# GpSimd's weight splits of a fused attention and MLP kernel, taken out from between four attention pairs and put behind them in larger groups

## Chip, cores and metric
The kernel runs on one core of a Trainium2 chip. The metric is the device time of one execution in microseconds (us). The time before is 1022.74 us, the median of 3 runs (1019.49 to 1027.27).

## What is computed
Attention over 4 batches, 8 heads, 576 positions, 64 channels, then two MLPs on the 2304 rows of 512 values that it gives. All data is float32.

```python
def _attn_ref(q, k, v):
    # downsampled by 4, softmax attention, repeated 4 times
    out_up = np.repeat(out_d, factor, axis=2)
    # local: |i - j| < 4
    scores = np.where(mask, scores, -1000000000.0)
    ...
    return (out_up + out_local).astype(np.float32)
def _moe_ref(x, w_in, w_out):
    h = x @ w_in
    g = h * np.cos(h)
    return (g @ w_out).astype(np.float32)
# then _moe2_ref: RMS norm, (silu(xn @ w_gate) * (xn @ w_val)) @ w_out
```

## The kernel before
**Work and its order.** Two heads form a pair, so that a batch has four attention pairs (PAIRS = 4). The rows are worked on in 6 chunks of 384. Batch 0's attention runs alone ("Wide", with several buffers); the attention of batches 1 to 3 ("Narrow", one buffer each) is spread by hand over the steps of the first MLP's chunks 0 to 2. Each engine has its own program, written out in order; they meet at semaphores.

**The first MLP and its weights.** A weight unit is a tile of 128x512 values. The first MLP has 32 of them (U1 = 32), the even ones for the product up (L984 to L986 with 384 columns), the odd ones for the product down (the same lines with 512 columns). TensorE multiplies in float32r; for accuracy each weight is split in a high part and the rest. ScalarE makes the high part of the first 16 units (U_EARLY = UP * PAIRS = 16, line L527, four after each pair of batch 0). GpSimd makes everything else: the high part of units 16 to 31 (L423) and the rest of all units (L425). Its function `split_unit` waits for the load, makes the high part if `hi_here` is true, waits for it, and makes the rest. Step f of a chunk on TensorE (`chunk1`, steps 0 to 18) needs unit 2f at its head for up(f) and unit 2(f - 3) + 1 for down(f - 3) later in the step.

**GpSimd's order.** For each pair j of batch 0: `value_sums` (sums of 4 rows of v: L399 and L404, once for each of the two heads), `normalise` twice (softmax times the reciprocal: L411 on the local part, L414 on the downsampled one), then four splits (units 4j to 4j + 3). Then `batch(1, (5, 5, 5, 1))`: for each pair of batch 1 the same sums and normalisations, and behind them 5, 5, 5 and 1 splits, units 16 to 31. Batches 2 and 3 have no splits.

**What waits for GpSimd.** TensorE's `transposes` of a pair (L937, L940) need `probs_ready`, which L414 gives. Its `values` (L953, L961) need `vd_ready` of L404. The next load of GpSimd's own operand, vg, stands in SyncE's queue behind a wait for `vd_ready`: the load for the second head of a pair is issued only when L404 of the first head is done. Behind it in the same queue stand the load of vw (L331), in pairs 0 and 1 of batch 1 that of a weight group (L335), and the load of the next pair's qk (L319).

**Places of batch 1's pairs on TensorE.** PE_WHERE gives, for each pair, the step and half of six pieces (scores of head 0, local scores of head 1, downsampled scores of head 1, transposes of head 0, of head 1, values). A half of 0 is behind up(step), one of 1 behind down(step - 3):

```python
    PE_WHERE = (((1, 0), (2, 0), (3, 0), (4, 0), (4, 1), (5, 0)),
                ((5, 1), (6, 0), (6, 1), (7, 1), (8, 0), (8, 1)),
                ((9, 0), (9, 1), (10, 0), (11, 1), (12, 0), (12, 1)),
                ((13, 0), (13, 1), (14, 0), (15, 0), (16, 0), (16, 1)))
```

**The other engines.** VectorE in batch 0: maxima and differences (L684, L691, L697, L699), sums and reciprocals (L710, L713, L717), copies of the transposed downsampled part (`copy_ptd`, L722), the four-row sums of q and k (L663), the addition of both attention parts into XY (`add_up`, L672). Before chunk 0, ScalarE copies a column third of x into the high part xs (L538) and VectorE makes its rest (L747). In the chunks VectorE has L779, L781, L787 and L751 for each f, ScalarE L570, L576, L578 and L547. On TensorE, the masks are L897 to L900, local scores L903, downsampled scores L920.

Of the kernel before, what the change touches and what calls it, by code (L numbers as in the profile page):

```python
# [31 lines left out]
U1, U2 = 2 * F1, 3 * F2  # L32
UP = 4
U_EARLY = UP * PAIRS
BANK = 12
GU = 4
QT = SD // 2
# [36 lines left out]
def attention_and_two_mlps(nc, qk, vwin, vgrp, w1, w2, rms_g, const, out):  # L74

    def at(name, shape, dtype, offset):
        return nc.alloc_sbuf_tensor_at(name, shape, dtype, offset=offset)
# [7 lines left out]

    W = [at(f"W{i}", [P, BANK, 2, 512], F32R, slots_at + i * BANK * 4096) for i in range(U2 // BANK)]
    W_raw = [at(f"W_raw{i}", [P, BANK, 2, 512], F32, slots_at + i * BANK * 4096) for i in range(U2 // BANK)]

# [37 lines left out]
    def part(start, end):  # L126
        small[:] = [start, end]
# [4 lines left out]
    buffers = {}  # L132
    for i, slot in enumerate((U1, 2 * BANK)):
        part(slots_at + slot * 4096, slots_at + (U2 if i == 0 else U1) * 4096)
# [54 lines left out]
    def loads(kind, b, j):  # L189

        return 1 if kind is Wide else PAIRS * b - PAIRS + j + 1
# [65 lines left out]
    def raw_of(bank, i):  # L257

        return W_raw[bank][:, bass.ds(i, 1), 1, :].rearrange("p o n -> p (o n)")

    def part_of(bank, i, part):

        return W[bank][:, bass.ds(i, 1), part, :].rearrange("p o n -> p (o n)")

    def group_of(bank, first):

        return W_raw[bank][:, bass.ds(first, GU), 1, :]

    def w_part(slot, part):
        return W[slot // BANK][:, slot % BANK, part, :]  # L270

# [5 lines left out]
    def y_tile(c, t):  # L277
        return XY[:, bass.ds(c * (TT * 512) + t * 512, 512)]
# [3 lines left out]
    def hold(eng, semaphore, value):  # L282

        eng.wait_ge(semaphore, value)
        if not isinstance(value, int):
            eng.sem_inc(passed, 1)
# [25 lines left out]
    def sync_program(sp):  # L313
# [13 lines left out]
        def load_values(kind, b, j):  # L327
            n = PAIRS * b + j
            if kind is Narrow:
                hold(sp, pv_done, n)  # L330
            sp.dma_start(kind.vw[j][:, :, :], vwin[bass.ds(n, 1)].rearrange("o p a d -> (o p) a d")).then_inc(kind.vw_in[j], 16)  # L331

        def load_group(src, g, slot0, k):

            sp.dma_start(group_of(slot0 // BANK, slot0 % BANK), src[GU * g:GU * g + GU].rearrange("u p n -> p u n")).then_inc(group_in[k], 16)  # L335

# [9 lines left out]
        load_values(Wide, 0, PAIRS - 1)  # L346
        for g in range(PAIRS - 1, 2 * BANK // GU):
            load_group(w1, g, GU * g, g)
# [33 lines left out]
    def pool_program(pool):  # L382
        g = nc.gpsimd
        g.memset(mhalf[:, :], -0.5).then_inc(setup, 1)
        g.memset(ones[:, :], 1.0).then_inc(setup, 1)

        g.memset(rinv[:, :], 1.0).then_inc(rinv_ready, 1)
        hold(pool, setup, 2)
        hold(pool, rinv_ready, 1)

        def value_sums(kind, b, j):

            n = PAIRS * b + j
            for s in range(2):
                vg = kind.vg[j][s]

                hold(pool, kind.vg_in[j], 32 if kind is Wide else 16 * (2 * loads(kind, b, j) - 1 + s))
                g.tensor_tensor(vg[0:QT, :, 0:2, :], vg[0:QT, :, 0:2, :], vg[0:QT, :, 2:4, :], ALU.add).then_inc(vt_ready, 1)  # L399
                hold(pool, vt_ready, 2 * n + s + 1)  # L400
                if kind is Narrow and s == 0:
                    hold(pool, pv_done, n)
                vd = kind.vd[j][:, :, :].rearrange("p (k s) d -> p k s d", s=2)[0:QT, :, s, :]
                g.tensor_tensor(vd, vg[0:QT, :, 0, :], vg[0:QT, :, 1, :], ALU.add).then_inc(vd_ready, 1)  # L404
                hold(pool, vd_ready, 2 * n + s + 1)

        def normalise(kind, b, j, s):
            u = 2 * (PAIRS * b + j) + s
            hold(pool, recip_ready, u + 1)
            p = kind.prob[j][:, s, 0:TP, :]  # L410
            g.tensor_tensor(p, p, recip[:, s, 0:TP].unsqueeze(2).to_broadcast([P, TP, WIN]), ALU.mult).then_inc(local_probs, 1)  # L411
            hold(pool, local_probs, u + 1)
            p = kind.probd[j][0:QT, s]
            g.tensor_tensor(p, p, recip[0:QT, s, TP:TP + 2].unsqueeze(2).to_broadcast([QT, 2, SD]), ALU.mult).then_inc(probs_ready, 1)  # L414
            hold(pool, probs_ready, u + 1)

        def split_unit(slot, order, hi_here=True):

            bank, i = divmod(slot, BANK)
            raw, hi, lo = raw_of(bank, i), part_of(bank, i, 0), part_of(bank, i, 1)  # L420
            hold(pool, group_in[order // GU], 16)
            if hi_here:
                g.tensor_tensor(hi, raw, ones[:, 0:1].to_broadcast([P, 512]), ALU.mult).then_inc(unit_hi, 1)  # L423
            hold(pool, unit_hi, order + 1)
            g.tensor_tensor(lo, raw, hi.bitcast(F32), ALU.subtract).then_inc(unit_ready, 1)  # L425
            hold(pool, unit_ready, order + 1)

        for j in range(PAIRS):
            value_sums(Wide, 0, j)  # L430
            normalise(Wide, 0, j, 0)
            normalise(Wide, 0, j, 1)
            for u in range(UP * j, UP * j + UP):
                split_unit(u, u, hi_here=False)

        def batch(b, units=(0,) * PAIRS):

            first = U_EARLY
            for j in range(PAIRS):
                value_sums(Narrow, b, j)  # L440
                normalise(Narrow, b, j, 0)
                normalise(Narrow, b, j, 1)
                for u in range(first, first + units[j]):
                    split_unit(u, u)
                first += units[j]
            scale_y(b - 1)

        def scale_y(c):

            hold(pool, ssq_ready, TT * c + TT)  # L450
            g.tensor_scalar(msq[:, :], ssq[:, :], 1.0 / DM, 1e-6, ALU.mult, ALU.add).then_inc(ms_ready, 1)
            hold(pool, ms_ready, c + 1)
            g.tensor_tensor(rinv[:, :], msq[:, :], mhalf[:, :], ALU.pow).then_inc(rinv_ready, 1)
            hold(pool, rinv_ready, c + 2)
            for t in range(TT):
                hold(pool, y_copied, TT * c + TT + t + 1)
                g.tensor_tensor(y_tile(c, t), y_tile(c, t), rinv[:, t:t + 1].to_broadcast([P, 512]), ALU.mult).then_inc(y_scaled, 1)

        batch(1, (5, 5, 5, 1))  # L460
        with pool.Fori(2, B) as b:
            batch(b)
        for u in range(GU):
            split_unit(U1 + u, U1 + u)
        with pool.Fori(ACH, NCH - 1) as c:
            scale_y(c)
        for u in range(U1):
            split_unit(u, U2 + u)
        scale_y(NCH - 1)
# [626 lines left out]
    with block as blk:  # L1096
        blk.sync(sync_program)
        blk.gpsimd(pool_program)
        blk.scalar(act_program)
        blk.vector(dve_program)  # L1100
        blk.tensor(pe_program)
# [52 lines left out]
```

## Time and profile before
| what | us |
|---|---|
| median of 3 runs (lowest, highest) | 1022.74 (1019.49, 1027.27) |
| span of the profiled execution | 1022.4 |
| TensorE busy | 991.5 (97%) |
| VectorE busy | 516.8 (51%) |
| ScalarE busy | 426.6 (42%) |
| GpSimd busy | 259.8 (25%) |

The page gives the profiled execution's span, from its first to its last instruction, and no device time of its own; the median of the three runs is 0.3 us above that span. In the rows, PE is TensorE, DVE VectorE, ACT ScalarE, POOL GpSimd and SP SyncE; L425 is line 425 of the kernel. "[0.25 <-DVE probd L722]" says that the engine sat idle for 0.25 us before the row and that VectorE's L722 ended this. PEclk is the granted clock as a share of full speed.

### The profile page before, as it was taken

What the parts mean: (1) busy time and instruction counts of PE and PEld (TensorE: products, weight loads), DVE (VectorE), ACT (ScalarE), POOL (GpSimd) and SP (SyncE); (2) the same over time, 40 slices, a digit from 0 to 9 for tenths busy, and PEclk for the clock granted to TensorE, in tenths of its full rate; (3) what the DMA queues carried; (4) which work ended last, traced back from release to release, by engine and by line L of the source; (5) the groups of instructions that cost most, each with busy time, mean ns of one, the idle gap of its engine ahead of it and who ended that gap; (6) DMA issues with size and microseconds to landing.
All of it is one profiled execution on the core that took longest, in us unless ns stands there. A gap on an engine that the chain in (4) does not pass through costs nothing.

```text
span 1022.4 us, 17445 instructions
## 1 busy us (share of the span) xinstructions
PE 991.5 (97%) x6320; PEld 887.3 (87%) x6320; DVE 516.8 (51%) x1176; ACT 426.6 (42%) x923; POOL 259.8 (25%) x285
## 2 busy tenths in 40 slices
PE   6889999999899999999999999999999999999998
PEld 5677787888788899998997999999999999999997
DVE  6767776676676664554667424324324324324322
ACT  3556566665665665655655213113113113112111
POOL 4947763221422150100299930000000000000000
PEclk9999999999999999999999999999999999999999
DMA  9622111111111100000134000000000000000000
GB/s 275 210 92 92 52 51 54 51 51 52 52 51 51 63 2 1 1 0 0 42 124 135 31 1 1 31 0 0 31 0 0 31 0 0 31 0 0 31 1 31
DMA packets 19208, 43.95 MB, mean 43 GB/s; under 512 B 1616, under 2 KB 1744, under 8 KB 19152
## 3 DMA queue, kind: packets, MB, share of 16 engines
q1 hardware_dynamic: 19152, 43.16, 12.9%
q8 instruction: 40, 0.66, 0.3%
q14 instruction: 16, 0.13, 0.0%
HBM read 38.44 MB, written 4.72 MB: 42 GB/s over the span
## 4 chain that ended last, share of the span: by engine, by line
PE 82%; DVE 6%; ACT 4%; POOL 3%; issue 3%; DMA 1%; DVEq 0%; SPq 0%; POOLq 0%; ACTq 0%
PE ps L984 26%; PE ps L986 25%; PE ps L985 25%; PE ps L903 2%; POOL W L425 1%; DVE ub L781 1%; ACT ub L576 1%; PE ps L920 1%; PE ps L1065 1%; DVE ub L779 1%; ACT ub L578 1%; DMA qk<-qk 1%; DVE XY L672 1%; ACT probd L487 1%; PE ps L937 1%
## 5 line engine op out<-in xcount | busy, mean ns | idle before, releaser
L984 PE MATMUL ps<-xs,W 128*128 128x384 f32 x960 | 327.8, 341 | 1.9 <-DVE xs L747 1.4
L986 PE MATMUL ps<-xs,W 128*128 128x384 f32 x960 | 324.0, 338 | 4.1 <-issue 4.1
L985 PE MATMUL ps<-xs,W 128*128 128x384 f32 x960 | 323.4, 337 | 0.0
L984 PE MATMUL ps<-W,ring 128*128 128x512 f32 x504 | 202.8, 402 | 0.0
L986 PE MATMUL ps<-W,ring 128*128 128x512 f32 x504 | 199.1, 395 | 0.0
L985 PE MATMUL ps<-W,ring 128*128 128x512 f32 x504 | 198.7, 394 | 0.0
L984 PEld LDWEIGHTS ps<-xs,W 128*128 128x128 f32 x960 | 181.4, 189 | 15.6 <-issue 7.6
L985 PEld LDWEIGHTS ps<-xs,W 128*128 128x128 f32 x960 | 181.6, 189 | 4.6
L986 PEld LDWEIGHTS ps<-xs,W 128*128 128x128 f32 x960 | 181.4, 189 | 0.0
L839 DVE TENSOR_TENSOR ub<-ub,ps 128x384 f32<-128x384 f32 x72 | 39.9, 554 | 248.9 <-ACT ub L629 248.9
L629 ACT ACTIVATE ub<-ps 128x384 f32<-128x384 f32 x72 | 35.4, 492 | 270.0 <-PE ps L986 270.0
L986 PEld LDWEIGHTS ps<-W,ring 128*128 128x128 f32 x504 | 94.9, 188 | 20.9
L984 PEld LDWEIGHTS ps<-W,ring 128*128 128x128 f32 x504 | 95.1, 189 | 18.6 <-issue 2.7
L985 PEld LDWEIGHTS ps<-W,ring 128*128 128x128 f32 x504 | 95.2, 189 | 15.8
L425 POOL TENSOR_TENSOR W<-W_raw,W 128x512 fp32r<-128x512 f32 x68 | 91.4, 1343 | 5.3
L787 DVE TENSOR_TENSOR ub<-ub,ps 128x384 f32<-128x384 f32 x96 | 53.0, 552 | 70.2 <-ACT ub L578 70.2
L570 ACT ACTIVATE ub<-ps,consts 128x384 f32<-128x384 f32 x96 | 55.1, 574 | 56.0 <-PE ps L986 54.2
L576 ACT ACTIVATE ub<-ub 128x384 f32<-128x384 f32 x96 | 50.4, 525 | 65.7 <-DVE ub L781 65.7
L635 ACT ACTIVATE ring<-ub 128x384 fp32r<-128x384 f32 x72 | 37.8, 525 | 82.6 <-DVE ub L843 82.6
L779 DVE TENSOR_SCALAR ub<-ub 128x384 f32<-128x384 f32 x96 | 44.7, 466 | 50.5 <-ACT ub L570 50.4
L848 DVE TENSOR_TENSOR ring<-ub,ring 128x384 fp32r<-128x384 f32 x72 | 42.7, 594 | 39.6 <-ACT ring L635 39.6
L751 DVE TENSOR_TENSOR ring<-ub,ring 128x384 fp32r<-128x384 f32 x96 | 60.9, 634 | 2.5 <-ACT ring L547 2.5
(91 smaller groups left out, 1014.5 us busy)
## 6 DMA issues: line engine op xcount, KB each, us to landing
W_raw<-w SPq DMA_DIRECT2D x17, 1024.0 KB, 6.1
qk<-qk SPq DMA_DIRECT2D x14, 576.0 KB, 4.1
vw<-vwin SPq DMA_DIRECT2D x14, 384.0 KB, 3.1
out<-XY SPq DMA_DIRECT2D x18, 256.0 KB, 2.0
vg<-vgrp SPq DMA_DIRECT2D x26, 144.0 KB
qk_more<-qk SPq DMA_DIRECT2D x2, 576.0 KB, 16.1
vg_more<-vgrp SPq DMA_DIRECT2D x6, 144.0 KB
vw_more<-vwin SPq DMA_DIRECT2D x2, 384.0 KB, 15.5
```

What stands on the lines that cost most here:

```text
L425: g.tensor_tensor(lo, raw, hi.bitcast(F32), ALU.subtract).then_inc(unit_ready, 1)
L570: a.activation(v, HB[f % NH], ACT.Identity, scale=INV_2PI, bias=consts[:, 0:1]).then_inc(turns_ready, 1)
L576: a.activation(v, v, ACT.Abs).then_inc(abs_ready, 1)
L635: a.activation(ring[:, f % 3, 0, :], ub[:, f % 2, :], ACT.Copy).then_inc(ahi_ready, 1)
L751: v.tensor_tensor(ring[:, f % 3, 1, :], ub[:, f % 2, :], ring[:, f % 3, 0, :].bitcast(F32), ALU.subtract).then_inc(glo_ready, 1)
L779: v.tensor_scalar(w, w, MAGIC, -2.0 * math.pi, ALU.subtract, ALU.mult).then_inc(angle0, 1)
L787: v.tensor_tensor(w, w, HB[f % NH], ALU.mult).then_inc(g_done, 1)
L839: v.tensor_tensor(w, w, GB[f % 2], ALU.mult).then_inc(silu_ready, 1)
L848: v.tensor_tensor(ring[:, f % 3, 1, :], w, ring[:, f % 3, 0, :].bitcast(F32), ALU.subtract).then_inc(alo_ready, 1)
L984: t_.matmul(dst, a_lo, b_hi, start=first, stop=False, skip_group_check=True)
L985: t_.matmul(dst, a_hi, b_lo, start=False, stop=False, skip_group_check=True)
L986: return t_.matmul(dst, a_hi, b_hi, start=False, stop=last, skip_group_check=True)
```

## The change
The four splits behind each pair of batch 0 are taken out of the loop over pairs. Behind the loop stand ten splits in a row, units 0 to 9 (U_FIRST = 10). Batch 1 starts at unit 10 and splits 8, 8, 6 and 0 units behind its pairs, where it split 5, 5, 5 and 1. The high part of units 10 to 15 still comes from ScalarE; GpSimd makes it from unit 16 on, as before. The number of splits, their operands and every other engine's program are the same.

```diff
+U_FIRST = 10
...
             value_sums(Wide, 0, j)
             normalise(Wide, 0, j, 0)
             normalise(Wide, 0, j, 1)
-            for u in range(UP * j, UP * j + UP):
-                split_unit(u, u, hi_here=False)
+        for u in range(U_FIRST):
+            split_unit(u, u, hi_here=False)
 
         def batch(b, units=(0,) * PAIRS):
 
-            first = U_EARLY
+            first = U_FIRST
             for j in range(PAIRS):
                 value_sums(Narrow, b, j)
                 normalise(Narrow, b, j, 0)
                 normalise(Narrow, b, j, 1)
                 for u in range(first, first + units[j]):
-                    split_unit(u, u)
+                    split_unit(u, u, hi_here=u >= U_EARLY)
                 first += units[j]
             scale_y(b - 1)
...
-        batch(1, (5, 5, 5, 1))
+        batch(1, (8, 8, 6, 0))
```

## Rows read from the trace of the kernel before

**Rows 1.** The page: busy time and share of each engine
```profile
PE 991.5 (97%) x6320; PEld 887.3 (87%) x6320; DVE 516.8 (51%) x1176; ACT 426.6 (42%) x923; POOL 259.8 (25%) x285
```

**Rows 2.** Chain that ended last, in order of time: start us, us, what
```profile
17.78 1.26 POOL W L425
...
48.85 0.67 POOL probd L414
```

**Rows 3.** Stretches: busy us of PE, PEld, DVE, ACT, POOL; PEclk, DMA share, GB/s
```profile
27.30:38.40 11.10, 10.73 (x116) 8.70 (x116) 9.12 (x26) 5.71 (x17) 10.19 (x12) 1.00 0.97 359
```

**Rows 4.** Timeline of TensorE, batch 0: start us, us, what, [idle before <-releaser]
```profile
31.65 0.87 PE L937 MATMUL ps<-ident,prob 128*128 128x128 f32 x3 [0.25 <-DVE probd L722]
...
46.60 1.23 PE L953 MATMUL ps<-probd,vd_more 72*64 72x144 f32 x8 [2.56 <-issue]
...
49.57 0.90 PE L937 MATMUL ps<-ident,prob 128*128 128x128 f32 x3 [0.28 <-POOL probd L414]
...
60.30 0.45 PE L984 MATMUL ps<-xs,W 128*128 128x384 f32 x1 [1.41 <-DVE xs L747]
```

**Rows 5.** Timeline of VectorE, batch 0
```profile
12.68 0.17 DVE L713 TENSOR_SCALAR sums<-sums 128x7 f32<-128x7 f32 x1
...
14.37 0.35 DVE L699 TENSOR_SCALAR dbias<-dmax 72x2 f32<-72x2 f32 x1
...
28.24 0.59 DVE L699 TENSOR_SCALAR dbias<-dmax 72x2 f32<-72x2 f32 x1
...
42.97 1.03 DVE L713 TENSOR_SCALAR sums<-sums 128x7 f32<-128x7 f32 x1
...
53.91 4.13 DVE L747 TENSOR_TENSOR xs<-XY,xs 128x384 fp32r<-128x384 f32 x3 [0.46 <-ACT xs L538]
...
59.69 0.56 DVE L747 TENSOR_TENSOR xs<-XY,xs 128x384 fp32r<-128x384 f32 x1 [0.59 <-ACT xs L538]
```

**Rows 6.** Timeline of GpSimd, batch 0 and pair 0 of batch 1
```profile
17.77 5.30 POOL L425 TENSOR_TENSOR W<-W_raw,W 128x512 fp32r<-128x512 f32 x4
...
51.13 5.49 POOL L425 TENSOR_TENSOR W<-W_raw,W 128x512 fp32r<-128x512 f32 x4
...
71.91 0.72 POOL L411 TENSOR_TENSOR prob<-prob,recip 128x320 f32<-128x320 f32 x1 [9.48 <-DVE recip L717]
```

**Rows 7.** Timeline of GpSimd, pairs 1 to 3 of batch 1
```profile
100.25 1.04 POOL L423 TENSOR_TENSOR W<-W_raw,ones 128x512 fp32r<-128x512 f32 x1
...
113.05 0.73 POOL L399 TENSOR_TENSOR vg<-vg 72x256 f32<-72x256 f32 x1
...
117.30 0.73 POOL L399 TENSOR_TENSOR vg<-vg 72x256 f32<-72x256 f32 x1 [2.60 <-DMA vg<-vgrp]
...
124.42 1.04 POOL L423 TENSOR_TENSOR W<-W_raw,ones 128x512 fp32r<-128x512 f32 x1
...
137.35 0.73 POOL L399 TENSOR_TENSOR vg<-vg 72x256 f32<-72x256 f32 x1
...
143.94 0.66 POOL L414 TENSOR_TENSOR probd<-probd,recip 72x288 f32<-72x288 f32 x1
```

**Rows 8.** Timeline of TensorE, chunk 0 and the start of chunk 1
```profile
79.13 0.42 PE L984 MATMUL ps<-xs,W 128*128 128x384 f32 x1
...
86.83 0.20 PE L897 MATMUL ps<-maskb,identb 128*128 128x64 bf16 x1 [1.46 <-DVE XY L672]
...
111.03 0.20 PE L897 MATMUL ps<-maskb,identb 128*128 128x64 bf16 x1 [1.33 <-DVE XY L672]
...
126.62 0.49 PE L937 MATMUL ps<-ident,prob 128*128 128x128 f32 x3
...
147.79 0.49 PE L937 MATMUL ps<-ident,prob 128*128 128x128 f32 x3
...
161.80 0.34 PE L986 MATMUL ps<-xs,W 128*128 128x384 f32 x1 [2.08 <-issue]
```

**Rows 9.** Stretches, columns as in rows 3: behind the first idle time of rows 8
```profile
88.00:92.00 4.00, 4.00 (x16) 3.77 (x15) 3.13 (x8) 2.87 (x6) 2.15 (x3) 0.59 0.16 41
```

## The prediction

> **What bounds the kernel now.** I read the page first. TensorE is busy for 991.5 of 1022.4 us [rows 1], so over most of the span only its own work sets the end. GpSimd is busy for 25% [rows 1], and the change touches only its order in the first 160 us. There I read the chain that ended last. From 17.78 to 49.5 us it runs through GpSimd without a gap, splits included [rows 2]. Taken alone this says that batch 0's attention is bound by GpSimd, and that its splits (1.26 us each and a gap of 0.08) are on the path.
>
> The busy times of one cycle, 27.3 to 38.4 us, say how much that is worth. In these 11.10 us GpSimd is busy for 10.19 and TensorE for 10.73 [rows 3]; TensorE's one idle time of size, 0.25 us, is ended by VectorE's L722 and not by GpSimd [rows 4]. So two engines are at their limit at once: GpSimd with some 5.75 us of attention and 5.36 us of splits a pair, TensorE with 10.8 us. Where two bounds stand 0.3 us apart, taking 5.36 us from one of them gives 0.3 us.
>
> **The change in batch 0.** What VectorE does beside a split is slower than alone: L713 takes 0.17 us alone and 1.03 beside one, L699 0.35 and 0.59 [rows 5]. Without the splits these come down. (a) In each of two full cycles L699 stands between TensorE's values of one pair and its next transposes: 0.25 us each, 0.5 us in all. (b) In the last cycle TensorE waited 2.56 us at L953 [rows 4] for the copy L722, which stands behind one L713 and one L699 more: 0.86 + 0.25 = 1.1 us less. (c) The next transposes waited 0.28 us for L414 [rows 4]; that goes. Sum: TensorE's transposes of pair 3 start at 49.57 - 1.9 = 47.65. Bounds: 0.3 us (if the sums and normalisations, which stay beside VectorE, slow it as much as the splits did) to 1.9 us; I take the latter, since rows 5 show both durations. GpSimd waits for VectorE's last reciprocal now (45.8) and is done with its last normalisation 1.5 us behind it, at 47.3 instead of 51.05.
>
> From there ten splits stand in a row: 10 x 1.34 = 13.4 us (four took 5.30, rows 6) and 0.3 more, until 61.0. In the kernel before, four stood there, and beside them the first three L747 took 4.13 us, where the fourth, alone, took 0.56 [rows 5]. The block is now long enough to cover the fourth too: 4.13 / 3 - 0.56 = 0.8 us on the path to TensorE's first full run. That run starts at 60.30 [rows 4]; after, at 60.3 - 1.9 + 0.8 = 59.2, 1.1 us earlier (0.5 later to 1.9 earlier by the bounds).
>
> The Trainium skill speaks against this placing: its page "SBUF — State Buffer", section "Who interferes with whom", says that a VectorE instruction with two SBUF inputs and a GpSimd instruction that reads SBUF exclude each other, so that the second fully waits. By that rule the fourth L747, which has two SBUF inputs, waits as the three did, and the sum below has its 0.8 us; without it the sum would be 0.8 us lower. The trace agrees for VectorE. It doesn't show GpSimd held in return: four splits with three L747 beside them took 5.49 us against 5.30 [rows 6].
>
> **Pair 0 of batch 1.** GpSimd sat idle for 9.48 us before L411 [rows 6], waiting for a reciprocal that follows from TensorE's chunk 0. The long block moves into that hole: value sums from 61.0, their second load and end at 66.8, the reciprocal at 70.8. So the normalisations come 1.1 us earlier like everything else. SyncE's queue, which waits for the first sum, issues vw and weight group 6 some 4 us later than before; values need the one behind up(5), splits the other at unit 24, both over 10 us later. Then 8 splits instead of 5. Six make only the rest (1.36 + 0.08 us, L425's mean there), two make both parts (2.56 us each: from 100.25 to 113.05 five take 12.80, rows 7): 8.7 + 5.1 = 13.8 us against 12.8. GpSimd gets to pair 1 at 88.7, which is about when it did. No split is late: up(5) needs unit 10 and starts at 79.13 [rows 8], after at 78.0; unit 10 is ready at 74.9 + 1.5 = 76.4, 1.6 us ahead. Later ones have more room: unit 30 is needed by up(15), at 145.7, and ready at 141.
>
> **Pairs 1 and 2: where it is paid.** Pair 1's splits started at 100.25 [rows 7], now at 99.1. Eight take 20.5 us instead of 12.8, to 119.6. The value sums of pair 2 start there instead of at 113.05, and their second load can't be asked for earlier, since it waits for the first sum: its 2.60 us [rows 7] stay. Sums 5.5 us (113.05 to 117.30 + 1.3), to 125.1; first normalisation 1.45, to 126.6. TensorE wants it for its transposes at 126.62 - 1.1 = 125.5 [rows 8]: it waits 1.1 us, and the whole lead is gone. Second normalisation to 128.2. Then six splits instead of five (124.42 to 137.35, rows 7: 2.58 each): 15.5 us, to 143.7. Value sums of pair 3 5.3 us, to 149.0; first normalisation 1.5, to 150.5. Before, that was done at 144.6 (143.94 + 0.66, rows 7), 3.2 us ahead of TensorE's transposes at 147.79 [rows 8]. Now TensorE, there at 147.8, waits 2.7 us. Queued behind these transposes are down(12), the second head's transposes, the values, and with them batch 1's x; TensorE can pass none of it. From 99.1 to 150.5 GpSimd alone is the bound, so that small shifts of TensorE in between are swallowed. Its last normalisation (152.1) is in time for the transposes at 153.3. The split taken from behind pair 3 frees only GpSimd, which waited there anyway.
>
> **The clock.** Two idle times of TensorE in chunk 0 (1.46 and 1.33 us, rows 8) were each followed by some 3.5 us at 1.2 GHz, the lower of its two levels: the granted clock of 88 to 92 us is 0.59 [rows 9], and matmuls of 384 columns start every 0.32 us instead of 0.173; 11 of them, 1.6 us lost. Two others (1.41 us before 60.30 in rows 4, 2.08 us before 161.80 in rows 8) weren't followed by one. So the new idle time of 2.7 us has an even chance of costing 1.6 us more: 0.8 us. The shorter one at 125.5 is covered by GpSimd's bound. Sum: 2.7 + 0.8 = 3.5 us. On the profiled span that is 1022.4 + 3.5 = 1025.9; the median of the runs stands 0.3 us above the span, and I say 1026.0. The unknown terms bound it from 2.0 us (no lower clock, GpSimd's run 0.7 us shorter) to 6.5 us (a lower stretch in pair 0 or 1, which moves 99.1 to 100.7, and another behind the wait): 1024.5 to 1029.
>
> **Rivals.**
> 1. Nothing to be seen (-1 to +1.5 us, 1022 to 1024.2). The lower clock of rows 9 may be gone, since all before it moves by 1 us; then GpSimd starts its 51.4 us 1.6 us earlier, and 2.7 becomes 1.1. Against the wait hiding of itself: 7.7 and 2.6 us of splits more stand against a room of 5.6 and 3.2 us at the two transposes, and GpSimd rests nowhere in that run but for its loads. Chance 0.15.
> 2. Faster. In batch 0 TensorE runs at 1.2 GHz: three L937 take 0.87 us there [rows 4] and 0.49 in chunk 0 [rows 8]. If the gaps close and the clock rises in batch 0, the cycle falls from 11.1 us to VectorE's 9.1 [rows 3], 2.0 us in each of three: 6.0 us, and 1020.0. It decides from 3.5 us on, a cycle under 9.9 us. Against it: TensorE was busy for 10.73 of 11.10 us and its clock didn't rise; 0.25 us less idle time is nearly the same picture. 0.09. That all three blocks of splits come off (3 x 5.36 = 16 us, 1010) needs TensorE to be no bound, against rows 3: 0.02.
> 3. Slower by more. Attention pieces that come late delay the MLP work of VectorE and ScalarE, TensorE idles, and the lower clock follows each time: three such stretches, 4.8 us, on top of 2.7: 1030.2. Against it: behind 150.5 little attention is left in this chunk, and batches 2 and 3 have no splits. 0.14.
>
> **How the numbers follow.** The forecast has 0.60, the rivals 0.15, 0.11 and 0.14. The range holds the forecast, rival 1, the first form of 2 and most of 3, with some room for the spread of single runs (7.8 us over three): 1019.5 to 1031. A change of 1%, 10 us, is about what a measurement of this kernel can tell from none. Faster by more needs rival 2's second form, 0.02; slower by more twice the loss of rival 3, 0.03; within 1% is 0.95.
>
> **What would show it.** In the profile after: TensorE's cycle in batch 0 still at 10.8 us or a little over; L713 near 0.2 us in it; ten L425 in a row from 47 to 61 us, and beside them four L747 of about 1.4 us; GpSimd's 9.5 us before L411 down to about 4; TensorE's first full run at 59.2; then idle time before L937, ended by GpSimd's L414, of 1 us near 126 and 2.7 us near 148. A cycle under 10 us in batch 0, or no wait of L937 for L414 in pairs 2 and 3, would make the forecast wrong; so would a TensorE that waits over 0.3 us at L984 for a split.

## The result, and the profile after

The changed kernel is slower by 0.4%: 1027.97 us against 1023.92 us (medians of 20 runs each), ratio 1.0042 with a 95% interval of 1.0029 to 1.0055, or 4.3 us (3.0 to 5.6); the two medians by themselves lie 4.05 us apart. The profiled execution went from 1022.4 to 1026.6 us. In the changed kernel each line behind L34 has a number higher by one: L425 is L426, L414 is L415, L937 is L938, L747 is L748.

The page, answering to [rows 1]:

```profile
PE 992.6 (97%) x6320; PEld 887.7 (86%) x6320; DVE 516.9 (50%) x1176; ACT 426.9 (42%) x923; POOL 259.6 (25%) x285
```

All busy times are those of before within 1.1 us: no work came or went; the 4 us are waiting and matmuls at the lower clock. The cycle of [rows 3], in the same columns:

```profile
27.30:38.40 11.10, 10.95 (x121) 8.99 (x120) 7.83 (x28) 5.86 (x18) 5.41 (x9) 1.00 0.91 339
```

GpSimd is busy for 5.41 us instead of 10.19, VectorE for 7.83 instead of 9.12 (its L713 and L699 no longer stand beside splits), and TensorE is still full: the second bound. Now the timeline of VectorE around chunk 0's start, answering to [rows 5], then of TensorE, answering to [rows 4] and [rows 8], then the granted clock of three stretches, columns as in rows 3.

```profile
51.09 4.38 DVE L748 TENSOR_TENSOR xs<-XY,xs 128x384 fp32r<-128x384 f32 x3 [0.46 <-ACT xs L539]
...
57.12 1.25 DVE L748 TENSOR_TENSOR xs<-XY,xs 128x384 fp32r<-128x384 f32 x1 [0.59 <-ACT xs L539]
...
60.12 0.96 DVE L780 TENSOR_SCALAR ub<-ub 128x384 f32<-128x384 f32 x1 [0.49 <-ACT ub L571]
```

```profile
58.42 0.44 PE L985 MATMUL ps<-xs,W 128*128 128x384 f32 x1 [2.10 <-DVE xs L748]
...
70.29 0.71 PE L921 MATMUL ps<-qkd 64*72 64x144 f32 x4 [0.44 <-ACT probd L488]
...
75.21 0.49 PE L938 MATMUL ps<-ident,prob 128*128 128x128 f32 x3
...
126.67 0.58 PE L938 MATMUL ps<-ident,prob 128*128 128x128 f32 x3 [2.58 <-POOL probd L415]
...
150.87 0.54 PE L938 MATMUL ps<-ident,prob 128*128 128x128 f32 x3 [1.24 <-POOL probd L415]
```

```profile
58.00:62.00 4.00, 3.58 (x12) 3.58 (x13) 3.15 (x4) 1.47 (x4) 3.73 (x4) 0.60 0.02 4
126.60:130.60 4.00, 3.93 (x17) 3.93 (x18) 1.47 (x3) 1.52 (x3) 3.74 (x4) 0.57 0.05 16
164.00:168.00 4.00, 3.21 (x11) 3.11 (x11) 2.58 (x3) 1.93 (x4) 3.22 (x5) 0.57 0.02 6
```

Executions differ in when their first loads land. I take GpSimd's first normalisation, which stands early in batch 0 behind these loads, as the mark of it: it began at 12.23 us here and at 13.23 us in the profile before, so 1.0 us of every "earlier" below comes with the execution and not with the kernel.

The fourth L748 grew from 0.56 to 1.25 us. TensorE's first full run came 1.9 us earlier, and from 58.9 us on ran at 1.2 GHz for 3.2 us (granted clock 0.60), so that pair 0's transposes stand at 75.21 where they stood at 75.31: the front gave nothing, and counted from the landing TensorE is 0.9 us later there. Then come the two waits for L415, 2.58 and 1.24 us, of which the kernel before had none. At 150.87 TensorE is 3.1 us behind [rows 8], 4.1 us counted from the landing; another 1.4 us come at 164 to 168, where this execution had the lower clock and the one before had not.

GpSimd's run between, answering to [rows 6] and [rows 7]:

```profile
60.95 0.73 POOL L400 TENSOR_TENSOR vg<-vg 72x256 f32<-72x256 f32 x1
...
71.79 0.72 POOL L412 TENSOR_TENSOR prob<-prob,recip 128x320 f32<-128x320 f32 x1 [5.70 <-DVE recip L718]
...
99.06 1.04 POOL L424 TENSOR_TENSOR W<-W_raw,ones 128x512 fp32r<-128x512 f32 x1
...
119.61 0.73 POOL L400 TENSOR_TENSOR vg<-vg 72x256 f32<-72x256 f32 x1
...
123.75 0.73 POOL L400 TENSOR_TENSOR vg<-vg 72x256 f32<-72x256 f32 x1 [2.86 <-DMA vg<-vgrp]
...
125.88 0.66 POOL L415 TENSOR_TENSOR probd<-probd,recip 72x288 f32<-72x288 f32 x1
...
128.17 1.42 POOL L424 TENSOR_TENSOR W<-W_raw,ones 128x512 fp32r<-128x512 f32 x1
...
150.07 0.66 POOL L415 TENSOR_TENSOR probd<-probd,recip 72x288 f32<-72x288 f32 x1
```

Eight splits, the sums with their load in between, two normalisations, six splits, sums, load, normalisation: 99.06 to 150.73 us without a rest but for the loads. TensorE starts again 0.1 us behind the ends of the two L415, 126.54 and 150.73.

### The profile page after: what moved, and what is told of

Read it like the earlier page. It is cut to its first block, busy times and chain, and to the rows that moved or that the text cites. A ratio compares the mean times of both kernels' runs of the same rounds, so it can differ in the third digit from the quotient of the medians.

```text
span 1026.6 us, 17445 instructions
## 1 busy us (share of the span) xinstructions
PE 992.6 (97%) x6320; PEld 887.7 (86%) x6320; DVE 516.9 (50%) x1176; ACT 426.9 (42%) x923; POOL 259.6 (25%) x285
## 4 chain that ended last, share of the span: by engine, by line
PE 80%; DVE 6%; POOL 4%; ACT 4%; issue 3%; DMA 2%; SPq 0%; DVEq 0%; ACTq 0%; POOLq 0%
PE ps L985 25%; PE ps L987 24%; PE ps L986 24%; POOL W L426 2%; PE ps L904 2%; POOL W L424 1%; DMA qk_more<-qk 1%; PE ps L921 1%; DVE ub L782 1%; ACT ub L577 1%; DVE XY L673 1%; PE ps L1066 1%; PE ps L962 1%; DVE ub L780 1%; ACT ub L579 1%
## 5 line engine op out<-in xcount | busy, mean ns | idle before, releaser
L426 POOL TENSOR_TENSOR W<-W_raw,W 128x512 fp32r<-128x512 f32 x68 | 91.8, 1351 | 5.3
L780 DVE TENSOR_SCALAR ub<-ub 128x384 f32<-128x384 f32 x96 | 45.2, 471 | 52.5 <-ACT ub L571 52.4
L752 DVE TENSOR_TENSOR ring<-ub,ring 128x384 fp32r<-128x384 f32 x96 | 61.4, 639 | 2.5 <-ACT ring L548 2.5
```

The source lines that it names most:

```text
L752: v.tensor_tensor(ring[:, f % 3, 1, :], ub[:, f % 2, :], ring[:, f % 3, 0, :].bitcast(F32), ALU.subtract).then_inc(glo_ready, 1)
L780: v.tensor_scalar(w, w, MAGIC, -2.0 * math.pi, ALU.subtract, ALU.mult).then_inc(angle0, 1)
```

## The experiments

Two theories. **A**: the added time is that run of GpSimd (the end), and the front is not free either, since splits beside VectorE's rests of x slow it. **B**, the rival: the added time comes from the front alone, the block of ten splits and the lower clock behind it; the late splits are hidden.

**One split moved from pair 2 to pair 3.**
```diff
-        batch(1, (8, 8, 6, 0))
+        batch(1, (8, 8, 5, 1))
```

> The changed kernel with one split moved from behind pair 2 of batch 1 to behind pair 3: 8, 8, 5, 1 instead of 8, 8, 6, 0. Theory A (the added time is GpSimd's run from pair 1's splits to pair 3's first normalisation, for which TensorE waits): that run ends 2.6 us earlier, TensorE's wait of 1.24 us before pair 3's transposes goes, that of 2.58 us before pair 2's stays, and the kernel is 1.2 to 2.8 us faster than the changed one: ratio to the kernel before 1.0015 to 1.003. Theory B (the added time comes from the front: the block of ten splits beside the rests of x, and the lower clock at 59 to 62 us): nothing moves, 1.004.

Measured 1.0034 (1.0017 to 1.005). TensorE in this kernel:
```profile
126.56 0.54 PE L938 MATMUL ps<-ident,prob 128*128 128x128 f32 x3 [2.39 <-POOL probd L415]
...
149.36 0.49 PE L938 MATMUL ps<-ident,prob 128*128 128x128 f32 x3
```
The second wait is gone, as A says, and the transposes of pair 3 come 1.5 us earlier than in the changed kernel. The time went down by 0.8 us, less than the 1.2 to 2.8 expected and inside the interval: the direction is A's, the ratio, which lies just above A's range, proves nothing alone.

**Old front, late end.**
```diff
 # the kernel before, four splits behind each pair of batch 0
-        batch(1, (5, 5, 5, 1))
+        batch(1, (2, 8, 6, 0))
```

> The kernel before with its four splits behind each pair of batch 0, but batch 1's splits as late as in the changed kernel: 2, 8, 6, 0. Theory A: GpSimd's run of 51.4 us starts at 100.2 as before, pair 3's first normalisation ends at 151.6 and TensorE is 3.8 us late at its transposes, perhaps 1.6 us more by a lower clock: ratio 1.0035 to 1.0055. Theory B: the front is the old one, so no difference, 1.000.

Measured 1.0034 (1.0015 to 1.0054), 3.5 us slower, just under A's 1.0035 to 1.0055. B falls: with the old front most of the loss is there. The two waits too:
```profile
123.92 0.54 PE L937 MATMUL ps<-ident,prob 128*128 128x128 f32 x3 [1.01 <-POOL probd L414]
...
147.83 0.54 PE L937 MATMUL ps<-ident,prob 128*128 128x128 f32 x3 [2.51 <-POOL probd L414]
```
The second start, 147.83, is that of the kernel before (147.79), but this execution's loads landed 1.8 us earlier, and the lower clock at 88 to 92 us, 1.6 us in the kernel before, wasn't there. With both taken into account it is some 3.4 us later. A lower clock follows the second wait (0.67 at 148 to 152).

**New front, old end.**
```diff
-U_FIRST = 10
+U_FIRST = 14
...
-        batch(1, (8, 8, 6, 0))
+        batch(1, (7, 5, 5, 1))
```

> The new front with the old end: no splits between batch 0's pairs, 14 in a row behind them, then 7, 5, 5, 1 in batch 1. Theory A: pair 1 and pair 2 have the splits of before, so TensorE waits nowhere for GpSimd in pairs 2 and 3, and the front's lead stays, 0.3 to 1.9 us: ratio 0.998 to 1.0000. Theory B: the block is longer still and covers the same rests of x, so the loss stays or grows: 1.004 or more.

Measured 1.0018 (1.0002 to 1.0035), between the two theories and in the range of neither. No wait for GpSimd is left in pairs 2 and 3:
```profile
69.98 0.71 PE L921 MATMUL ps<-qkd 64*72 64x144 f32 x4 [1.46 <-ACT probd L488]
...
76.45 0.49 PE L938 MATMUL ps<-ident,prob 128*128 128x128 f32 x3
...
127.96 0.49 PE L938 MATMUL ps<-ident,prob 128*128 128x128 f32 x3
...
149.13 0.49 PE L938 MATMUL ps<-ident,prob 128*128 128x128 f32 x3
```
But the lead that A still gave to the front isn't there; this front costs 1.8 us (0.2 to 3.6). TensorE's first full run came at 57.09, and ten of its matmuls ran at the low clock, one every 0.32 us; then L921 waited 1.46 us for ScalarE. That wait was 0.44 us in the changed kernel: the block here has 14 splits and not ten, runs until 65.0 and so stands beside more of chunk 0 (L700 took 1.10 us), so the 1.8 us can't be taken as the cost of the changed kernel's own front. With the 3.5 us of the late end it makes 5.3, where the whole change costs 4.3; the intervals, some 2 us to either side, allow both.

**Sums between the splits.** The next three ask what the block beside the rests of x is worth.
```diff
 # with U_FIRST = 14 and (7, 5, 5, 1) of the run above
-        for u in range(U_FIRST):
+        for u in range(UP):
             split_unit(u, u, hi_here=False)
+        value_sums(Narrow, 1, 0)
+        for u in range(UP, U_FIRST):
+            split_unit(u, u, hi_here=False)
 # and pair 0 of batch(1) makes no value sums
```

> As the run with 14 splits in a row and 7, 5, 5, 1 behind them, but batch 1's first value sums stand behind the first four of the 14. GpSimd then waits some 4 us (for the values of pair 3 and the second load) where VectorE makes the rests of x. Theory A with contention as priced: of four L747 at most one or two are slow, TensorE's first full run starts 1.5 to 3 us earlier than in the changed kernel's 58.4, and the ratio is 0.996 to 0.999. Theory B (front alone): the front's cost goes too, 1.000 or below. If splits beside the rests of x cost nothing, it equals the run with 14 in a row.

Measured 0.9994 (0.9978 to 1.001): 2.4 us less than with 14 in a row by the two ratios, though the intervals overlap a little. From the start of the first rest of x to the end of the fourth it takes 4.97 us instead of 7.29.

**The same in the changed kernel alone** (U_FIRST = 10, then 8, 8, 6, 0).

> The changed kernel with one thing moved: batch 1's first value sums stand behind the first four of the ten splits. The end is the changed kernel's 8, 8, 6, 0. Theory A: the rests of x end 2.3 us earlier, the lower clock at 59 to 62 us is gone, so GpSimd's run of 51.4 us starts 2 to 4 us earlier, and so does the end: ratio 1.000 to 1.002 instead of 1.004. Theory B (only the late run matters): 1.004.

Measured 1.0021 (1.0004 to 1.0037), half of the loss, just outside what A expected (1.002) and nearer to it than to B's 1.004. The two waits stand nearly in full (2.48 and 1.13 us) and TensorE starts behind the second one at 148.34, 2.5 us ahead of the changed kernel (0.5 of it the landing), so the gain is the front's: GpSimd's late run started earlier. And VectorE shows where the gain stopped (here L752 is L747, L784 is L779, L704 is L699, L756 is L751):
```profile
50.00 2.76 DVE L752 TENSOR_TENSOR xs<-XY,xs 128x384 fp32r<-128x384 f32 x3 [0.46 <-ACT xs L543]
...
57.10 1.45 DVE L784 TENSOR_SCALAR ub<-ub 128x384 f32<-128x384 f32 x1 [0.87 <-ACT ub L575]
...
61.19 1.25 DVE L704 TENSOR_SCALAR dbias<-dmax 72x2 f32<-72x2 f32 x1
...
62.82 1.17 DVE L784 TENSOR_SCALAR ub<-ub 128x384 f32<-128x384 f32 x1
...
64.49 1.07 DVE L756 TENSOR_TENSOR ring<-ub,ring 128x384 fp32r<-128x384 f32 x1
```
The splits left the rests of x and now stand beside chunk 0's first steps, and 0.36, 0.17, 0.36 and 0.55 us became 1.45, 1.25, 1.17 and 1.07. TensorE waited 2.15 us for ScalarE's L487 behind them.

**Both, with a balanced end** (4 splits, sums, 8 splits, then 7, 6, 6, 1).

> Front: no splits between batch 0's pairs, then 4 splits, batch 1's first value sums, 8 splits. End: 7, 6, 6, 1 splits behind batch 1's pairs. Theory A (two parts: the block beside the rests of x costs 2.3 us and brings a lower clock worth 1.6 us; GpSimd's late run in pairs 1 to 3 costs some 3 us): neither is left, TensorE's first full run starts near 55 us at an early landing of the loads, no wait of L938's successor for GpSimd over 0.3 us in pairs 2 and 3; ratio 0.996 to 0.998. Theory B (only the late run matters, the block costs nothing): 0.999 to 1.000, as the front's lead alone would give 1 us or less.

Measured 1.0001 (0.9983 to 1.002). The waits did as A said (0.33 us before pair 3's transposes, none before pair 2's), and chunk 1's first run went on at 157.25 where the kernel before had 161.80 (1.2 us of it the landing); but the time is that of the kernel before, and A's 0.996 to 0.998 is a miss. In its profile the span behind that point is 4.8 us longer than before. Two lower clocks stand there that the kernel before had not, the first worth 1.4 us, the second at most 1.7 (columns as in rows 3):
```profile
157.00:161.00 4.00, 3.75 (x15) 3.64 (x15) 2.33 (x3) 2.07 (x3) 3.84 (x5) 0.66 0.03 6
...
552.00:556.00 4.00, 2.79 (x11) 2.32 (x12) 3.50 (x10) 1.14 (x4) 3.77 (x4) 0.78 0.70 255
```
The rest of the 4.8 us is not assigned.

**Old front, sums ahead of the last four splits.**
```diff
 # the kernel before
+            if j == PAIRS - 1:
+                value_sums(Narrow, 1, 0)
             for u in range(UP * j, UP * j + UP):
                 split_unit(u, u, hi_here=False)
 # and pair 0 of batch(1) makes no value sums
```

> The kernel before with one thing moved: batch 1's first value sums stand ahead of the four splits behind batch 0's last pair. These four then run in the hole of 9.5 us before batch 1's first normalisation and not beside the rests of x. Theory A: the first three L747 take 1.7 to 2.8 us instead of 4.1, TensorE's first full run starts 1.4 to 2.4 us earlier, ratio 0.9975 to 0.999. Theory B (splits beside the rests of x cost nothing in the end): 1.000.

Measured 1.0005 (0.9988 to 1.0022): no gain. In the profile (L750 is L747, L782 is L779, L702 is L699, L923 is L920):
```profile
52.50 1.50 DVE L750 TENSOR_TENSOR xs<-XY,xs 128x384 fp32r<-128x384 f32 x3 [0.46 <-ACT xs L541]
...
59.60 1.32 DVE L782 TENSOR_SCALAR ub<-ub 128x384 f32<-128x384 f32 x1 [0.86 <-ACT ub L573]
...
63.52 1.29 DVE L702 TENSOR_SCALAR dbias<-dmax 72x2 f32<-72x2 f32 x1
```
```profile
69.52 0.71 PE L923 MATMUL ps<-qkd 64*72 64x144 f32 x4 [1.37 <-ACT probd L490]
```
The three rests of x took 1.50 us instead of 4.13, and the fourth ended 1.1 us earlier than in the run with the old front and the late end (57.47 and 58.54), though the loads landed 0.4 us later (11.79 and 11.43). Two things took these 1.5 us back. TensorE, which now had no wait for x, ran 12 matmuls at the lower clock where it ran six there, about 0.8 us. And L779 and L699, beside the four splits, became 1.32 and 1.29 us, and TensorE's wait at L920 behind them 1.37 us instead of 0.24.

**Splits in the hole, nothing else.** This isolates what GpSimd's idle 9.48 us of [rows 6] are worth.
```diff
 # the kernel before; high_part is the first half of split_unit
                 value_sums(Narrow, b, j)
+                if isinstance(b, int) and j == 0:
+                    for u in range(U_EARLY, U_EARLY + 8):
+                        high_part(u, u)
                 normalise(Narrow, b, j, 0)
...
-                    split_unit(u, u)
+                    split_unit(u, u, hi_here=u >= U_EARLY + 8)
```

> The kernel before with the high parts of units 16 to 23 made early, eight L423 in a row in the hole ahead of batch 1's first normalisation; pair 0's five splits and three of pair 1's are then rests only. 
Measured 1.001 (0.9995 to 1.0024): the time alone shows no difference. The clean reading is in two profiles whose loads landed alike (11.43 and 11.44), so that both stand at 58.59 at TensorE's first full run. VectorE and TensorE with an empty hole (the run with the old front and the late end), then with eight high parts in it, 8.58 us from 60.83 on (L707 is L699, L787 is L779, L759 is L751, L928 is L920, L945 is L937):
```profile
63.82 0.17 DVE L699 TENSOR_SCALAR dbias<-dmax 72x2 f32<-72x2 f32 x1
...
64.36 0.35 DVE L779 TENSOR_SCALAR ub<-ub 128x384 f32<-128x384 f32 x1
...
65.22 0.55 DVE L751 TENSOR_TENSOR ring<-ub,ring 128x384 fp32r<-128x384 f32 x1
```
```profile
68.70 0.71 PE L920 MATMUL ps<-qkd 64*72 64x144 f32 x4 [0.24 <-ACT probd L487]
...
73.62 0.49 PE L937 MATMUL ps<-ident,prob 128*128 128x128 f32 x3
```
```profile
63.82 1.07 DVE L707 TENSOR_SCALAR dbias<-dmax 72x2 f32<-72x2 f32 x1
...
65.27 0.93 DVE L787 TENSOR_SCALAR ub<-ub 128x384 f32<-128x384 f32 x1
...
66.71 0.81 DVE L759 TENSOR_TENSOR ring<-ub,ring 128x384 fp32r<-128x384 f32 x1
```
```profile
70.19 0.71 PE L928 MATMUL ps<-qkd 64*72 64x144 f32 x4 [1.73 <-ACT probd L495]
...
75.08 0.49 PE L945 MATMUL ps<-ident,prob 128*128 128x128 f32 x3
```
Three instructions grew by 0.90, 0.58 and 0.26 us, 1.7 in all, and TensorE is 1.5 us later at both of its lines. The hole isn't free; what of the 1.5 us reaches the end of the kernel is not shown.

**Three splits a pair.** What the findings suggest: GpSimd out of TensorE's way in batch 0, few splits beside chunk 0's start, an end without waits.
```diff
 # the kernel before
+            if j == PAIRS - 1:
+                value_sums(Narrow, 1, 0)
-            for u in range(UP * j, UP * j + UP):
+            for u in range(3 * j, 3 * j + 3):
                 split_unit(u, u, hi_here=False)
...
-        batch(1, (5, 5, 5, 1))
+        batch(1, (7, 6, 6, 1))
 # batch 1 starts at unit 12, and its pair 0 makes no value sums
```

> Three splits behind each pair of batch 0 instead of four, the first value sums of batch 1 ahead of the last three, then 7, 6, 6, 1. GpSimd has 5.75 + 4.0 us in a cycle of batch 0, less than TensorE's 10.8, so it is no bound; only three splits stand in the hole. Theory A: the front's lead is 2 us or more at the rests of x, of which contention in the hole takes 0.5 us; pairs 2 and 3 wait for GpSimd 0.3 us at most: ratio 0.997 to 0.999. If the lead is taken back by other waits of chunk 0, 1.000.

Measured 0.9986 (0.997 to 1.0001). Once more:

> Three splits behind each pair of batch 0, sums ahead of the last three, then 7, 6, 6, 1, timed once more, since the first interval (0.997 to 1.0001) just reaches 1. Theory A: 0.9985 again, 1.5 us faster. Theory B (no different from the kernel before): 1.000.

Measured 0.9989 (0.997 to 1.0008). Both are 1.1 to 1.4 us faster, both intervals reach 1.

**A fourth split behind the last pair.** The same with four splits behind batch 0's last pair, then 7, 6, 5, 1.

> The same with a fourth split behind batch 0's last pair, and 7, 6, 5, 1 in batch 1. GpSimd's run to pair 3's first normalisation is 2.6 us shorter, so that the wait of 1.2 us before pair 3's transposes goes; one split more in the hole costs VectorE up to 0.5 us. Theory A: ratio 0.997 to 0.999, at least as fast as with three. If the wait was worth nothing, the same as with three.

Measured 0.9996 (0.9974 to 1.0019). The wait before pair 3's transposes is gone and TensorE goes on in chunk 1 at 156.99, 1.4 and 0.8 us ahead of the two profiles with three, but the time isn't lower. No version is shown to beat the kernel before; the one with three splits a pair is the best candidate.

**The changed kernel again.**

> The changed kernel, profiled once more. Of the changed kernel itself (not of the execution) are: ten splits in a row, 7.3 us from the first L748 to the end of the fourth, a lower clock at TensorE's first full run, a wait for GpSimd before the transposes of pairs 2 and 3 whose ends stand 75 to 78 us behind pair 1's last normalisation less the loads. Of the execution may be: the landing of the first loads (up to 2 us) and where else the clock falls.

A span of 1025.0 us, from a single run. TensorE's waits:
```profile
126.59 0.54 PE L938 MATMUL ps<-ident,prob 128*128 128x128 f32 x3 [0.56 <-POOL probd L415]
...
150.50 0.54 PE L938 MATMUL ps<-ident,prob 128*128 128x128 f32 x3 [2.50 <-POOL probd L415]
```
Their ends are those of the first profile (126.67, 150.87) within 0.4 us, though the waits are shared out otherwise (0.56 and 2.50 against 2.58 and 1.24). Here TensorE had the lower clock at 88 and 112 us, as in the kernel before, and came to the first wait later. So in these two profiles the ends belong to the kernel and the length of each wait to the execution. The loads landed 0.3 us earlier than in the first profile (GpSimd's first normalisation at 11.95 against 12.23; in the kernel before 13.23). My expected distance of 75 to 78 us between the waits and pair 1's last normalisation was a slip: it is 27 and 51 us.

## Why the prediction was right

The forecast was 3.3 us above the median known then; measured are 4.3 us (3.0 to 5.6). The main mechanism, GpSimd's late run, is as predicted; the front was not, and its error was partly hidden by luck. By its steps:

- **Batch 0, 1.9 us earlier.** Transposes of pair 3 stand at 46.68, 2.9 us before 49.57, and 1.0 us of that is the loads' earlier landing: 1.9 us. The two bounds 0.3 us apart hold too: GpSimd's first normalisations of a pair follow each other in 10.8 and 10.7 us, where they took 11.1. One reading of [rows 5] was wrong: L699's 0.35 us is not its time alone. It stands beside a normalisation (L414); alone L699 takes 0.17 us, at 65.53 in the kernel before. The sum was not hurt, since the normalisations stay, and L699 took 0.30 to 0.35 us in batch 0's cycles after. The gain was larger in other executions. From GpSimd's first normalisation to the first rest of x it took 40.7 us in the kernel before and 40.7 to 40.8 in the three others with four splits a pair, whenever the loads landed; with no splits between it took 38.0 to 38.9.
- **The block.** Ten splits took 14.2 us (predicted 13.7), the fourth rest of x 0.7 us more (0.8), TensorE's first full run 0.9 us earlier net of the landing (1.1). Right.
- **The front's lead of 1.1 us.** Wrong in what follows: I let it run through to 99.1, and it was gone by pair 0's transposes (75.21 and 75.31). The clock took most of it. The prediction had no lower clock at TensorE's first full run; here ten matmuls ran at it, 1.5 us, and L921 waited 0.2 us longer, with L780 ahead of it at 0.96 us instead of 0.36. In the three profiles where TensorE's wait for x was 2.1 us (this one, the one with a split moved back, the one with 14 splits in a row) the clock had risen before the wait and fell again right behind it; in the three with waits of 1.1 to 1.4 us (the kernel before and two runs with its block of four) it had risen too and stayed. The second profile of the changed kernel waited 1.6 us, its clock had not risen before, and eight matmuls behind the wait ran at the lower one. "The long block moves into that hole" cost nothing in my sum either; how much it costs depends on how far the splits reach into chunk 0: 0.2 us at L921 here, 1.5 us with the eight in the hole.
- **Pair 0.** GpSimd's idle time fell to 5.70 us (I said about 4), it reached pair 1 at 89.8 (88.7), no split was late. Pair 1's splits start at 99.06 (99.1), since the 1.6 us of lower clock at 88 to 92 in [rows 9] wasn't there this time and the loads had landed 1.0 us earlier. That this number fits is luck.
- **GpSimd's run.** Predicted 51.4 us from 99.1, with normalisations done at 126.6 and 150.5; measured 51.7 us, 126.54 and 150.73. The waits were to be 1.1 and 2.7 us, together 3.8; they were 2.58 and 1.24, together 3.8, and 0.56 and 2.50 in the second profile. TensorE behind them: 2.7 us late predicted, 3.1 measured, or 4.1 counted from the landing, because the run, counted so, began at 100.1 and not at 99.1, and was 0.3 us longer. This run is the term that carries the forecast, and the run with the old front and the late end shows it without the new front: 3.5 us (1.5 to 5.5).
- **The clock, 0.8 us.** A lower clock followed the first wait (126.6 to 130.6, swallowed by GpSimd's run as foreseen) and not the second; one more at 164 to 168 cost 1.4 us in this profile and wasn't in the other of the same kernel. Two profiles can't show that 0.8 was a fair mean. Over all profiles the even chance was low for a wait of that length: behind the five waits for GpSimd of 2.4 to 2.6 us in chunk 0 a lower clock followed in four, behind the eight of 0.3 to 1.3 us in none.
- **The sum.** The steps give 1022.74 + 3.5 = 1026.2, not 1026.0, and the two terms of the upper bound 5.9 us, not 6.5. Nothing hangs on either. That 1% is the least that can be told was too pessimistic: with 20 runs each, 0.4% is clear.
- **Rivals.** Rival 2, a higher clock in batch 0, did not occur: GpSimd's first normalisations, one a cycle, stand at 20.59, 31.40 and 42.12. Rival 1 had the lower clock of 88 to 92 gone, which happened in one of two profiles, but the wait didn't shrink with it, since the front had used the lead up. Of rival 3's stretches one more came than before (three in the first profile, 58 to 168 us, against two), and one of the three was swallowed.

## What to carry to other kernels

When an engine works between two of its own deadlines, add up its run from the last thing it must wait for to the next thing others wait for, loads in its way included; if work moved into that run is longer than the room at its end, the difference is paid, wherever the work came from. And an idle stretch of GpSimd wasn't free room here: what stands there runs beside another stretch of VectorE, and the price moves along with the work. A lead won early is worth what is left of it at the next meeting point, so follow it there before it enters the sum.

## What the runs showed of the hardware

- GpSimd's splits lengthen short VectorE instructions of two kinds, whose operands all lie in SBUF. TENSOR_SCALAR: L699 with 2 elements a partition from 0.17 to 1.07 and 1.29 us, L779 from 0.35 to 1.45. TENSOR_TENSOR with two SBUF inputs: L751 from 0.55 to 1.07, L747 from 0.56 to 1.25. Not every one: the reciprocal L717 takes 0.20 us beside a split (at 32.92 in the kernel before) and without one. GpSimd loses little: ten splits in 14.21 us beside four L748, where 13.4 would be their time alone. The Trainium skill's page "SBUF — State Buffer", section "Who interferes with whom", names both kinds of VectorE instruction and says that tensor_reduce never contends on trn2; the trace agrees (in the kernel before, L663 takes 1.34 us at 28.75 beside a split and 1.35 at 60.17 without one). It also says that whoever comes second is held for the whole instruction. VectorE's times fit that. GpSimd's don't: four L748 of 0.56 us, each holding the next split but for the gap of 0.08, would cost it 1.9 us, and it lost 0.8.
- An earlier start of TensorE's work can be paid back by its clock. In the changed kernel with the sums between the splits TensorE's first run of the MLP had no wait at all, from 52.24 us on, and 14 of its matmuls ran at the lower clock, one every 0.32 us; in the kernel before 5 did, ahead of its wait for x. The column PEclk doesn't show this: it reads 1.00 in 27.30:38.40, and up to 56 us in every profile, though three L937 take 0.87 us there and 0.49 in chunk 0. Up to its first change the durations tell the clock.
- The landing of the first loads moves batch 0 by up to 1.9 us between executions (GpSimd's first normalisation at 11.35 to 13.23 us over 14 profiles), and a lower clock of some 3.5 us stood at the start of chunk 1 in 10 of the 13 other profiles and not in that of the kernel before, whose wait there (2.08 us) was of the same kind as theirs (2.0 to 2.7). What decides this one stays open; it is as large as the gains sought here.
